# Fused attention and two mixers: channel weights of the second mixer split later, z's low part before the tile's, and a third block at the last pair's first product

## The reference

```python
def _moe2_ref(x, w_theta, w_tok_r, w_tok_i, w_ch):
    theta = x @ w_theta
    cos_t, sin_t = (np.cos(theta), np.sin(theta))
    zr = x * cos_t
    zi = x * sin_t
    yr = np.einsum('ts,bsd->btd', w_tok_r, zr)
    yi = np.einsum('ts,bsd->btd', w_tok_i, zi)
    y = yr + yi
    u = x + y
    return (u + np.maximum(u @ w_ch, 0.0)).astype(np.float32)
```

## Time and profile before

| | us |
|---|---|
| median of 3 runs | 496.13 |
| profiled execution, own time | 497.82 |
| span of its records | 496.00 |
| TensorE busy (matmuls) | 487.6 |
| DVE busy | 325.8 |
| POOL busy | 267.7 |
| ACT busy | 192.3 |

### The profile page before, as it was taken

One profiled execution on the slowest core, in us unless ns is written; L12 is line 12 of the kernel. 1 busy time (PEld: TensorE's weight loads), 2 busy tenths in 40 slices (PEclk: granted clock), 3 DMA queues, 4 the chain that ended last, 5 costly groups with the idle time before them and its releaser, 6 DMA issues.

```text
span 496.0 us, 8394 instructions
## 1 busy us (share of the span) xinstructions
PE 487.6 (98%) x2917; PEld 445.6 (90%) x2917; DVE 325.8 (66%) x797; ACT 192.3 (39%) x413; POOL 267.7 (54%) x315
## 2 busy tenths in 40 slices
PE   7999999999999999999999999999989999999997
PEld 5999999899999999889999998888878899888897
DVE  7998999569535433399625436798887665655552
ACT  6999898555112121146112214344232321321230
POOL 3575566599798983739798882554930310000040
PEclk9999999999999999999999999999989999999999
DMA  7897675522132232104242242133102211000002
GB/s 239 326 304 242 239 219 147 157 85 84 58 95 85 83 110 85 44 0 128 64 129 85 72 134 72 65 110 125 42 2 60 67 66 64 0 1 0 2 32 96
DMA packets 27083, 49.81 MB, mean 100 GB/s; under 512 B 3360, under 2 KB 17696, under 8 KB 27040
## 3 DMA queue, kind: packets, MB, share of 16 engines
q1 hardware_dynamic: 27040, 49.26, 31.6%
HBM read 39.81 MB, written 3.15 MB: 87 GB/s over the span
## 4 chain that ended last, share of the span: by engine, by line
PE 87%; DVE 11%; issue 1%; ACT 1%; DMA 1%; DVEq 0%
PE bank L323 63%; PE bank L1800 7%; PE bank L1506 5%; PE bank L1536 4%; PE bank L1539 4%; PE bank L1520 2%; PE bank L1518 2%; DVE act_raw L1224 2%; DVE zc L1240 1%; DVE zs L1258 1%; DVE act_raw L1218 1%; DVE za L1234 1%; DVE tile L1202 1%; DVE zb L1253 1%; DMA counts<-both_counts 1%
## 5 line engine op out<-in xcount | busy, mean ns | idle before, releaser
L323 PE MATMUL bank<-wsplit 128*128 128x256 f32 (+2 forms) x816 | 148.8, 338 | 0.0
L323 PEld LDWEIGHTS bank<-wsplit 128*128 128x128 f32 x816 | 134.1, 188 | 13.3
L710 POOL TENSOR_TENSOR wsplit<-wraw,wsplit 128x512 fp32r<-128x512 f32 (+1 forms) x77 | 102.1, 1327 | 41.4 <-ACT wsplit L883 25.5
L323 PE MATMUL bank<-wsplit,zs 128*128 128x512 f32 (+1 forms) x576 | 105.0, 342 | 2.1 <-DVE zs L1258 2.1
L323 PEld LDWEIGHTS bank<-wsplit,zs 128*128 128x128 f32 x576 | 90.9, 191 | 16.7 <-issue 2.5
L778 POOL TENSOR_TENSOR split<-act_raw,split 128x384 fp32r<-128x384 f32 x12 | 12.5, 1079 | 105.5 <-ACT split L1008 105.5
L652 POOL TENSOR_TENSOR wsplit<-qk_raw,wsplit 64x256 fp32r<-64x256 f32 x46 | 38.0, 827 | 33.1 <-DVE wsplit L1051 32.8
L323 PE MATMUL bank<-split,wsplit 128*128 128x384 f32 x276 | 53.8, 339 | 0.4 <-DVE zb L1235 0.3
L704 POOL CAST wsplit<-wraw 128x512 fp32r<-128x512 f32 (+1 forms) x59 | 36.1, 612 | 26.9 <-PE bank L323 17.5
L323 PEld LDWEIGHTS bank<-split,wsplit 128*128 128x128 f32 x276 | 47.3, 188 | 1.1 <-DVE zb L1235 0.5
L1371 DVE SCALAR_TENSOR_TENSOR wsplit<-bank,wsplit 128x384 fp32r<-128x384 f32 x30 | 16.7, 558 | 38.1 <-ACT wsplit L961 26.9
(11 more groups left out here) (126 smaller groups left out, 749.9 us busy)
## 6 DMA issues: line engine op xcount, KB each, us to landing
wraw<-weights SPq DMA_DIRECT2D x28, 512.0 KB, 3.4
qk_raw<-qk SPq DMA_DIRECT2D x23, 528.0 KB, 4.5
wraw<-weights SPq DMA_DIRECT2D x8, 768.0 KB, 4.1
vt<-v SPq DMA_DIRECT2D x10, 520.0 KB, 4.6
xT<-turned SPq DMA_DIRECT2D x64, 48.0 KB, 2.0
out<-act_raw SPq DMA_DIRECT2D x16, 192.0 KB, 1.9
xT<-turned_early SPq DMA_DIRECT2D x16, 96.0 KB, 2.7
xT<-wraw SPq DMA_DIRECT2D x32, 48.0 KB, 2.0
```

What stands on the lines that cost most here:

```text
L323: mm = pe.matmul(dst, lhs(a), rhs(c), start=first and i == 0, stop=last and i == 2, skip_group_check=True)
L710: ins = pool.tensor_tensor(dst[:, cols], src[:, cols], hi[:, cols].bitcast(F32), ALU.subtract)
```

## The change

It has three edits. CHAN_FROM goes from 3 to 5, so POOL waits for 5 and 7 finished half steps, in place of 3 and 5, before it splits the two chunks of channel weights. In the token mixing DVE makes the low part of z's first half (`z_to_lo(g, 0)`) in front of the low part of the x tile (`tile_to_lo`), not behind it. And in the last pair TensorE runs three blocks behind the angles of tile 0, not two; the blocks behind them move up by one, so that one block instead of two stands behind the last product.

```diff
@@ -71,7 +71,7 @@
 MIX_RAW_AT = RING1_AT + 2 * RING1
 TOKRI_AT = [4, 2, 3, 5, 8, 6]
 CHAN_AT = [7, 9]
-CHAN_FROM = 3
+CHAN_FROM = 5
 LAST_BANK = [[0, 1, 2, 3, 0, 1, 2, 3], [6, 7, 0, 1, 2, 3, 6, 7]]
 HALF = 1024
 QUAD = 32
@@ -1429,10 +1429,10 @@
                     if g >= 2 and not (b and s == 0):
                         find_angles(g)
                         multiply_x(g)
+                    if g >= 2 and not (b and s == 0):
+                        z_to_lo(g, 0)
                     if g >= 2 and g + 2 < B * T:
                         tile_to_lo(B * T + g + 2)
-                    if g >= 2 and not (b and s == 0):
-                        z_to_lo(g, 0)
                     if g == 2:
                         for i in range(3, 2 * KD):
                             finish_x2(B - 1, i)
@@ -1696,8 +1696,8 @@
                     ahead = b == B - 1 and i == PAIR_F - 1
                     if ahead:
                         angles(0)
-                        block(i - 1, *blocks[0])
-                        block(i - 1, *blocks[1])
+                        for at in range(3):
+                            block(i - 1, *blocks[at])
                         pe.wait_ge(th_taken, 1)
                     wait_weight(pair_in_order(b, i, 0))
                     pe.wait_ge(r1_lo, parts - 1)
@@ -1706,18 +1706,18 @@
                         first_block(0, *blocks[0], 2)
                         first_block(0, *blocks[1], 2)
                     else:
-                        block(i - 1, *blocks[2 if ahead else 0])
+                        block(i - 1, *blocks[3 if ahead else 0])
                     pe.wait_ge(p1_copied, m + 1)
                     product(i, 1, 6, quarter(2, 0), True)
                     if i == 1:
                         rest_of_block(0, *blocks[0])
                         rest_of_block(0, *blocks[1])
                     else:
-                        block(i - 1, *blocks[3 if ahead else 1])
+                        block(i - 1, *blocks[4 if ahead else 1])
                     pe.wait_ge(r1_lo, parts)
                     pe.wait_ge(t_lo, b * SUMS + 6)
                     product(i, 4, 7, summed(2), False)
-                    block(i - 1, *blocks[4 if ahead else 2])
+                    block(i - 1, *blocks[5 if ahead else 2])
                     pe.wait_ge(r1_lo, parts + 1)
                     product(i, 5, 6, summed(3), False)
                     if not ahead:
@@ -1729,10 +1729,11 @@
                     pe.wait_ge(u_taken, 3 * m + 2)
                     pe.wait_ge(t_lo, b * SUMS + 8)
                     product(i, 2, 6, summed(4), False)
-                    block(i - 1, *blocks[5])
+                    block(i - 1, *blocks[6 if ahead else 5])
                     pe.wait_ge(u_taken, 3 * m + 3)
                     product(i, 6, 7, quarter(2, 1), True)
-                    block(i - 1, *blocks[6])
+                    if not ahead:
+                        block(i - 1, *blocks[6])
                     block(i - 1, *blocks[7])
 
                 if b == B - 1:
```

## The result

The changed kernel took 498.93 us (median of 7 runs, 497.51 to 499.87) beside 496.19 for the kernel before in the same comparison (496.01 to 497.76). The ratio is 1.0044, with a 95% interval of 1.0027 to 1.0062 (the quotient of the two medians alone would be 1.0055). The forecast was 494.7, with a range of 493.4 to 496.3. The kernel is slower by less than 1%, and the difference is clear of noise.

What follows compares the result with a forecast made beforehand. TensorE, busy 98%, was taken as the bound, leaving its waits and one slow-clock slice to win. +0.55 - 1.23 - 1.47 + 0.72 = -1.43 us, put onto the median 496.13, gave 494.7, range 493.4 to 496.3.

Steps and rivals of the forecast that it cites:

- The 1.47 us of the clock: Half step 6 (first half of token tile 3): the clock no longer falls behind its shortened wait, -1.47 us.
- +0.55 - 1.23 + 0.72: Later token mixing from the third block, shorter wait at half step 6, new wait at half step 10, in us.
- edit 3: Token mixing, z's low part before the x tile's: DVE idles 0.18 us; half step 6 starts 1.23 us earlier, with CHAN_FROM 5.
- Edit 1: Last pair, third block before the wait for tile 0's angles: TensorE gains 0.53, yet all engines come 0.55 us later.
- the bank 6 wait: Last pair, tile 1's angles: TensorE waits 0.67 us until DVE has taken the third result part from bank 6.
- Edit 2: CHAN_FROM 5: channel weight chunk 1 moves from step 3 to step 4, costing a new 0.72 us wait at half step 10.
- The wait left at half step 6: First half of token tile 3: some 1.05 us of weight loads, 0.88 us of matmuls, without a clock fall.
- Chunk 0: First channel weight chunk on POOL: doesn't move, as POOL is busy until 354.04 anyway; worth 0.
- the holding looks shorter: DVE/POOL port lock: DVE waited at most 1.09 us for POOL operations taking 1.48, so not held the whole instruction.
- the upper end of the range: 496.3 us, given for the clock falling at half step 10 (sum +0.04, time 496.2).
- (c): Rival: chunk 1 in step 4 moves the 2.1 us wait, clock included, to half step 10; +1.43, 497.6 us; chance 0.10 with other slower cases.

Runs made afterwards that it cites:

- Edit 3 alone: Kernel before with only z's low part put in front of the x tile's low part: ratio 1.0074, median 499.73 us.
- the idle alone: Kernel before in its old order, plus one DVE wait for ACT's high part of z in step 2 (0.18 us idle): ratio 1.0049, median 499.97 us.
- edit 1 alone: Kernel before with only the third block at the last pair's first product: ratio 1.0013, 496.55 us with the clock up.
- edit 3 from step 3 on: Kernel before with z's low part in front of the x tile's from step 3 on, old order in step 2: ratio 0.9971, 495.88 us clock up.
- the later turning: Kernel before with CHAN_FROM 5, z's low part first from step 3 on, and DVE turning all six x tiles behind step 5: ratio 0.9956.
- the kernel before once more: The kernel before, unchanged, run and profiled again: median 496.28 us, ratio 1.0002.
- the last version: Kernel before with CHAN_FROM 7, z's low part first from step 3 on, x turned behind step 5, POOL waiting for z's low part (2,1): ratio 0.9941.

## Why the prediction was wrong

**The base.** The step that failed first is "a difference within the kernel should be the same in both, so I put the change onto the median". The 1.47 us of the clock were in the profiled execution (half step 6 took 5.82 us in it and 4.29 where the clock stayed up) and not in the median of the runs. The sum should have read that the 1.69 us by which the profile lay above the median had a place: the fallen clock is 1.5 of it, the longer wait 0.1. A median without the fall can't win it. Without that term the sum is +0.55 - 1.23 + 0.72 = +0.04, no change, and that is what the changed kernel with the old order in step 2 measured: 496.22 beside 496.18.

**The race.** The second step that failed is in edit 3: "So DVE idles 0.18 us in step 2. That is handed down by DVE to step 3, and POOL's chunks go with it, because its first operation there waits for DVE." That first operation starts when ACT releases it; it waited for DVE only because DVE had got in first, and 0.18 us decide that. For the same reason "DVE operations with two inputs in SBUF and POOL's operations alternate" doesn't hold in the trace it was read from: one operation of POOL stood behind four of DVE there. The step counts 0.18 and it costs 3.3 us on DVE; on TensorE it is a wait of 2.94 us at the angles of tile 4 less the 2.18 us at half step 6. Edit 3 alone and the idle alone show it, and undoing it in step 2, or holding POOL back, takes it away.

The miss of 4.2 us adds up: 1.5 for the base (494.7 to 496.22), 1.65 for the lost race (to 497.87, the median with the clock up) and 1.1 for the fall of the clock in most runs (to 498.93). With the clock up the changed kernel took 497.51 to 497.91 (three of seven runs), 1.3 to 1.7 us more than before; its trace with a fall, against the trace of before with a fall, has the half steps from 7 on 1.12 us later (371.21 against 370.09). The rest of the 2.7 us between the medians is how often the clock fell: in four of seven runs of the changed kernel.

**What was right.** Edit 1: the bank 6 wait of 0.67 (measured 0.65), all engines 0.55 later at token mixing (0.46 on TensorE and 0.47 on DVE in the trace, 0.51 in the time of edit 1 alone). The block took 1.01 us and not 1.08, so that the loads behind it came 0.48 later (301.03 against 300.55). Beyond that the traces don't settle the slide: at tile 2's product with x DVE was 0.2 us later (344.71 against 344.50), and there the kernels without edit 1 lie up to 0.5 apart among themselves. Edit 2: 0.72 us of new wait at half step 10 (0.70 alone, 0.74 with all edits but step 2), and behind it 2.2 us lost by DVE to POOL in step 4 (2.16 measured in the latter: the products zc and zb took 1.76 and 1.78 us for 0.69 each). The wait left at half step 6: 1.05 forecast, 1.07 measured, in the kernel with the old order in step 2. That the clock doesn't fall behind a wait of this size: it was up in 9 of 10 runs. Chunk 0, costed as unmoved, was so only while DVE won: in the changed kernel POOL was done early and waited 0.54 us for half step 4.

**Two readings beside the sum.** The 1.48 us for an operation of POOL is the mean of three, and the later two had themselves waited for DVE. The first took 1.30, so DVE's longest wait of 1.09 us is close to a whole operation, and "the holding looks shorter" rests on 0.2 us and not on 0.4. And the upper end of the range, 496.3, is given for a case that its own sum puts at 496.2.

**The rivals.** None had the place. (c) had the mechanism, DVE waiting for POOL's operations one after the other until an old wait has moved and taken the clock along, and came within 1.3 us of the time (497.6), but it put it into step 4 with the moved chunk, and gave it 0.10. The slower side deserved more: the profile had one operation L710 of POOL in step 2 that stood still beside DVE, in the 6.12 us for three where others took 4.43, and the prediction passes over it.

**What stays open.** Which instant decides the race. DVE won in seven traces with POOL's operation 0.127 to 0.134 us behind the start of the third L1224. POOL won at 0.122 behind it, at 0.055 to 0.058 before it (three traces), and at 0.27 us inside another 512-column operation. From the end of the second L1224 the winning and the losing case are both 0.04 to 0.05 us away, so the instants in the traces don't separate them. Why a wait of about 2 us lets the clock fall in some executions and not in others isn't settled either. The runs of before near 499 have no trace, but their mean clock speaks for two falls and a race that was won: one fall takes the mean from 1.000 to 0.996 or 0.997 and costs 1.5 us, and they stand at 0.992 to 0.993 and about 3 us above. A kernel with a lost race and a mean clock of 0.993 took 500.6 (the idle alone).

## What to carry to other kernels

Before a profile is used as the base of a sum, set its own time against the runs' median: a gap of 1.7 us in a kernel whose three runs agree within 0.2 is an event in that execution, and what it shows there may not be winnable. Where two engines can hold each other up, the order in which they come is a state that a shift of 0.2 us can flip; look for an operation that stands still far beyond its usual time, and ask what happens if the other one wins. Such a race can be taken out with a wait on the engine that is off the path. Here that wait made nothing faster by itself; the 1.9 us against the kernel before came with CHAN_FROM 7, edit 3 from step 3 on and the later turning, which took work of POOL and DVE out of TensorE's way, and the wait kept them from being lost to the race, in six runs out of six.

## What the runs showed of the hardware

A stream of back-to-back DVE operations with two SBUF inputs can keep an operation of POOL out for 1.7 us (POOL's L710 took 2.98 us for 1.29 alone), while a POOL operation that gets in once makes the next three DVE operations wait about 1.1 us each (1.5 to 1.8 us for 0.42 to 0.69). In one program the winner can change from one execution to the next; this rests on one slow execution that has a trace, beside four faster ones that have none.

How long TensorE's matmuls stood still doesn't alone decide whether the clock falls. Behind 2.00 us without a matmul the granted clock stayed at 1.00 (the kernel before once more); behind 2.11 (the kernel before) and 1.89 (edit 1 alone) it fell to the lower level (1.2 GHz), and that costs 1.5 us. Over many runs the longer wait has more falls. By the longest gap between weight loads in the profiled execution: 49 of 90 runs of the kernel before at about 2.2 us (from 12 of 29 to 22 of 31 by comparison), 5 of 12 at 2.06, 7 of 31 at 1.30 to 1.48 (three kernels), 1 of 10 at 1.07, 1 of 8 at 0.99, none of 6 at 0.54 (the last version). In the four kernels that lost the race in their traces (the changed one, edit 3 alone, the idle alone, the other order of x2's pieces), at 2.9 to 4.3, it was 27 of 33.
